# First two heads of a fused attention and MLP kernel: the ranking of head 1 before score 0, one inverse for three tiles, v of head 0 later

## What is computed

```python
q_assign = np.argmax(np.einsum('bhsd,hcd->bhsc', q_n, c_n), axis=-1)
k_assign = np.argmax(np.einsum('bhsd,hcd->bhsc', k_n, c_n), axis=-1)
mask = q_assign[:, :, :, None] == k_assign[:, :, None, :]
scores = np.where(mask, scale * np.matmul(q, k.transpose(0, 1, 3, 2)), -1000000000.0)
attn = np.exp(scores - np.max(scores, axis=-1, keepdims=True))
attn = attn / (np.sum(attn, axis=-1, keepdims=True) + 1e-09)
x = np.matmul(attn, v)
...
g = P / (Q + 1e-06)
x2 = g @ w_out
...
out = silu(x2 @ w_gate) * (x2 @ w_val) @ w_out
```

## Time and profile before

| what | value |
|---|---|
| median of 3 runs | 784.21 us (783.18 to 785.2) |
| the profiled execution's own time | 783.12 us |
| its span in the profile | 781.4 us, so 1.72 us lie around it |
| PE busy | 775.7 us (99%) |
| DVE, ACT, POOL busy | 569.3, 514.9, 524.8 us |
| DMA queue of SP and ACT (q1) | 27.0% of 16 engines |

### The profile page before, as it was taken

The page is one execution under the profiler, slowest core; times in us unless marked ns, Lnnn a source line. Parts: engine busy times, 40 slices in busy tenths (PEclk is TensorE's granted clock), DMA queues, the critical chain, the costliest instruction groups (busy, mean ns, idle before and its releaser), DMA issues.

```text
span 781.4 us, 12694 instructions
## 1 busy us (share of the span) xinstructions
PE 775.7 (99%) x4239; PEld 702.2 (90%) x4239; DVE 569.3 (73%) x1046; ACT 514.9 (66%) x958; POOL 524.8 (67%) x459
## 2 busy tenths in 40 slices
PE   9999999999999999999999999999999999999998
PEld 9999999999998888888888888899999999999997
DVE  6999999999996888777776877654544555554454
ACT  5888888888886787777768789554544444333322
POOL 6778999998585898212222488879888975665620
PEclk9999999999999999999999999999999999999999
DMA  8775674644302600000000011342111204211002
GB/s 196 172 189 147 173 175 120 162 120 117 85 29 82 189 0 1 1 0 1 1 0 1 28 30 53 87 131 54 48 34 55 55 27 136 55 37 46 27 1 81
DMA packets 57521, 57.53 MB, mean 74 GB/s; under 512 B 6576, under 2 KB 44272, under 8 KB 57456
## 3 DMA queue, kind: packets, MB, share of 16 engines
q1 hardware_dynamic: 57216, 56.13, 27.0%
q10 hardware_dynamic: 240, 0.59, 0.3%
HBM read 33.59 MB, written 3.15 MB: 47 GB/s over the span
## 4 chain that ended last, share of the span: by engine, by line
PE 98%; DVE 1%; ACT 0%; issue 0%; POOL 0%; ACTq 0%; POOLq 0%
PE ps L1247 19%; PE ps L1249 19%; PE ps L1248 19%; PE ps L1399 8%; PE ps L1416 4%; PE ps L1343 4%; PE ps L1344 4%; PE ps L1342 4%; PE ps L1418 4%; PE ps L1380 4%; PE ps L1385 4%; PE ps L1450 3%; PE ps L1243 1%; DVE probT_lo L1169 0%; PE ps L1354 0%; DVE neg_max L1143 0%
## 5 line engine op out<-in xcount | busy, mean ns | idle before, releaser
L570 POOL TENSOR_TENSOR den<-den,mag 128x512 f32<-128x512 f32 x48 | 62.3, 1298 | 122.0 <-ACT den L759 121.8
L629 POOL TENSOR_TENSOR w_lo<-w_raw,w_hi 128x768 fp32r<-128x768 f32 (+1 forms) x48 | 101.7, 2127 | 56.4 <-ACT w_hi L812 56.4
L1249 PE MATMUL ps<-x_hi,w_lo 128*128 128x512 f32 (+1 forms) x384 | 139.4, 363 | 0.0
L1247 PE MATMUL ps<-x_hi,w_hi 128*128 128x512 f32 (+1 forms) x384 | 139.1, 362 | 0.0
L1248 PE MATMUL ps<-x_lo,w_hi 128*128 128x512 f32 (+1 forms) x384 | 139.1, 362 | 0.0
L656 POOL TENSOR_SCALAR prob<-prob,row_inv 128x768 f32<-128x768 f32 x96 | 85.6, 907 | 29.3 <-DVE row_inv L1159 28.2
L1169 DVE TENSOR_TENSOR probT_lo<-ps,probT_hi 128x384 fp32r<-128x384 f32 x192 | 97.5, 549 | 6.5 <-ACT probT_hi L900 5.5
L900 ACT ACTIVATE probT_hi<-ps 128x384 fp32r<-128x384 f32 x192 | 83.7, 488 | 26.1 <-PE ps L1399 24.9
L1143 DVE TENSOR_REDUCE neg_max<-ps 128x1 f32<-128x768 f32 x96 | 90.9, 948 | 1.0 <-PE ps L1385 0.8
L880 ACT ACTIVATE prob<-ps,neg_max 128x768 f32<-128x768 f32 x96 | 86.7, 903 | 1.5 <-DVE neg_max L1143 1.2
L1399 PE MATMUL ps<-ident,prob 128*128 128x128 f32 x576 | 80.1, 275 | 1.3 <-DVE probT_lo L1169 1.1
(11 more groups left out here) (150 smaller groups left out, 1994.3 us busy)
## 6 DMA issues: line engine op xcount, KB each, us to landing
w_raw<-in_moe_w_gate SPq DMA_DIRECT2D x48, 128.0 KB, 2.3
w_raw<-in_moe_w_val SPq DMA_DIRECT2D x48, 128.0 KB, 2.6
k_hihi<-qk_hi SPq DMA_DIRECT2D x31, 192.0 KB, 4.0
w_raw<-in_moe_w_in SPq DMA_DIRECT2D x16, 256.0 KB, 3.6
w_raw<-in_moe_w_out SPq DMA_DIRECT2D x16, 256.0 KB, 4.9
qk_raw<-in_q SPq DMA_DIRECT2D x16, 192.0 KB, 3.3
qk_low<-qk_hi SPq DMA_DIRECT2D x16, 192.0 KB, 4.4
v_raw<-in_v SPq DMA_DIRECT2D x16, 192.0 KB, 2.6
```

The source lines that it names most:

```text
L629: did(g.tensor_tensor(lo[:, wave, :], raw[:, wave, :], hi[:, wave, :].bitcast(F32), ALU.subtract), s_w2lo)
L1247: mm(dst, hi, m_hi, start=start, stop=False)
L1249: return mm(dst, lo, m_hi, start=False, stop=stop)
```

## The change

Head 1's table now has both groups of logits at steps -10 and -9, the sum, the largest and the marks at -8 and -7, the transposed marks at -6, and rank and cluster rows at -5, all ahead of score 0 at step 0. `marks_at` needs no exception for head 1 any more, and ACT's cluster rows of head 0 (L956) go behind the copy of head 1's marks (they now stand at the step of head 1's cluster rows, -5). SP's order of DMAs is the same but for v of head 0, which is loaded behind the six small DMAs of head 1's cluster rows. POOL splits it at step 5 in place of -4; the low part of head 3 moves from step 5 to 4. `den_at` has no single tiles any more: the three tiles of the first half get one sum and one reciprocal, at step 3, behind the marks of head 2 (`last`). The zeros behind head 0's marks go from 5 to 4; the 4 and 7 beside head 1's logits go, and 3 come behind head 1's transposed marks; ahead of score 4 there are 2, not 3; ahead of turn 1 there are 2, not 4.

```diff
--- before.py
+++ after.py
@@ -266,12 +266,12 @@
     STAGES = (0, 2, 8, 8, 8, 8, 10, 10, 11, 11)
     FIRST = {S_LOGIT_0: -12, S_LOGIT_1: -11, S_SUM: -10, S_TOP: -10, S_MARKS: -9, S_TOPT: -8, S_RANK: -7, S_CLUSTER: -6}
     FOURTH = {S_LOGIT_0: 6, S_LOGIT_1: 7}
-    SECOND = {S_LOGIT_0: -10, S_LOGIT_1: -7, S_SUM: -6, S_TOP: -6, S_MARKS: -5, S_TOPT: 1, S_RANK: 2, S_CLUSTER: 2}
+    SECOND = {S_LOGIT_0: -10, S_LOGIT_1: -9, S_SUM: -8, S_TOP: -8, S_MARKS: -7, S_TOPT: -6, S_RANK: -5, S_CLUSTER: -5}
     THIRD = {S_SPLIT: -5, S_LOGIT_0: 2, S_LOGIT_1: 3, S_SUM: 3, S_TOP: 3, S_MARKS: 3, S_TOPT: 4, S_RANK: 5, S_CLUSTER: 6}
-    FIRST_V, FIRST_W1, LOW_AT = -4, 5, {3: 5, 4: 9}
-    FIRST_DEN, FIRST_T, FIRST_PV = 2, 4, 8
-    WARM_CEN, WARM_CENT, WARM_LOGIT, WARM_MARKS, WARM_TOP, WARM_ROWS, WARM_TILE = 19, 6, 4, 4, 5, 7, 3
-    WARM_TURN, WARM_RANK = 4, 2
+    FIRST_V, FIRST_W1, LOW_AT = 5, 5, {3: 4, 4: 9}
+    FIRST_T, FIRST_PV = 4, 8
+    WARM_CEN, WARM_CENT, WARM_LOGIT, WARM_TOP, WARM_NEXT, WARM_TILE = 19, 6, 4, 4, 3, 2
+    WARM_TURN, WARM_RANK = 2, 2
     STEPS = range(FIRST_STEP, NT + PV_LAG + HALF + 1)
 
     def head_at(step, stage):
@@ -303,7 +303,7 @@
 
     def marks_at(step):
 
-        return 1 if step == 0 else head_at(step, S_RANK) if head_at(step, S_RANK) != 1 else None
+        return head_at(step, S_RANK)
 
     def turn_at(step):
 
@@ -313,10 +313,8 @@
 
     def den_at(step):
 
-        if FIRST_DEN <= step < FIRST_DEN + HALF:
-            return 0, slice(step - FIRST_DEN, step - FIRST_DEN + 1)
         half = (step - HALF) // HALF
-        if (step - HALF) % HALF == 0 and 1 <= half < NG:
+        if (step - HALF) % HALF == 0 and 0 <= half < NG:
             return half, slice(half % 2 * HALF, half % 2 * HALF + HALF)
         return None, None
 
@@ -457,11 +455,11 @@
             load_qk(1)
             load_qk(2)
             copy_hi(0, hi_copies(0))
-            load_v(0)
             load_qk(3)
             copy_hi(1, hi_copies(1))
             copy_lo(1)
             send_cluster(1)
+            load_v(0)
             load_qk(4)
             copy_hi(2, hi_copies(2))
             copy_lo(2)
@@ -651,7 +649,7 @@
             for step in STEPS:
                 half, cols = den_at(step)
                 if half is not None:
-                    pool.wait_ge(s_inv, HALF + half if half else cols.stop)
+                    pool.wait_ge(s_inv, half + 1)
                     for i in range(cols.start, cols.stop):
                         did(g.tensor_scalar(prob[i][:, :], prob[i][:, :], row_inv[:, i:i + 1], 1.0,
                                         ALU.mult, ALU.mult), s_norm)
@@ -676,7 +674,7 @@
                     if step == when:
                         split_low(h)
 
-                h = (step - V_STEP) // T if step > 0 else 0
+                h = (step - V_STEP) // T if step >= T else 0
                 if step == (T * h + V_STEP if h else FIRST_V) and h < NH:
                     pool.wait_ge(s_v_in[h % 2], 16 * (h // 2 + 1))
                     if h >= 2:
@@ -950,7 +948,7 @@
                 h = early_at(step, S_SUM)
                 if h is not None:
                     copy_low(h)
-                if early_at(step, S_CLUSTER) == 0:
+                if early_at(step, S_CLUSTER) == 1:
 
                     sc.wait_ge(s_row0, 2)
                     s.activation(qk_low[0][0:C, 0, :].rearrange("c (t n) -> c t n", t=T)[:, 1:T, :],
@@ -1147,15 +1145,14 @@
                 half, cols = den_at(step)
                 if half is not None:
 
-                    n = HALF + half if half else cols.stop
                     if half >= 2:
                         ve.wait_ge(s_norm, HALF * (half - 1))
                     else:
                         ve.wait_ge(s_eps, 1)
-                    ve.wait_ge(s_exp, HALF * (half + 1) if half else cols.stop)
+                    ve.wait_ge(s_exp, HALF * (half + 1))
                     v_.tensor_reduce(row_den[:, cols], row_sum[:, cols, :], AX.X, ALU.add
                                      ).then_inc(s_den, 1)
-                    ve.wait_ge(s_den, n)
+                    ve.wait_ge(s_den, half + 1)
                     v_.reciprocal(row_inv[:, cols], row_den[:, cols]).then_inc(s_inv, 1)
 
             def low_parts(step):
@@ -1193,7 +1190,8 @@
                     marks(h)
                 maximum(step)
                 late = step >= 2 * T and step % T == HALF
-                if not late:
+                last = step == HALF
+                if not late and not last:
                     inverses(step)
                 if products_first(step):
                     x_sum(step)
@@ -1218,6 +1216,8 @@
                 h = early_at(step, S_MARKS)
                 if h is not None:
                     marks(h)
+                if last:
+                    inverses(step)
                 if step == 4 * T:
                     ve.wait_ge(s_par_in, 32)
                     v_.tensor_scalar(a_neg, a_raw, -1.0, None, ALU.mult)
@@ -1354,8 +1354,8 @@
                     last = transpose(ps[0:T * C, PREP, n * P:(n + 1) * P],
                                      is_top[:, n, :, :].rearrange("p t c -> p (t c)"), ident[:, :])
                 last.then_inc(s_topT, 1)
-                if h == 0:
-                    warm(WARM_TOP)
+                if h < 2:
+                    warm((WARM_TOP, WARM_NEXT)[h])
 
             def scores(step):
                 i = tile_at(step)
@@ -1454,10 +1454,6 @@
                     last.then_inc(s_logit, 1)
                     if h == 0:
                         warm(WARM_LOGIT)
-                    elif h == 1:
-                        warm(WARM_ROWS)
-                elif h == 1:
-                    warm(WARM_MARKS)
 
             pe.wait_ge(s_zeros, 1)
             warm(WARM_CEN)
```

## The result

| | before | after |
|---|---|---|
| median | 783.99 us (783.18 to 785.75, 17 runs) | 785.49 us (784.41 to 787.46, 17 runs) |
| profiled execution, its span | 783.12, 781.4 us | 785.49, 783.7 us |
| start of turn 0, start of turn 2 on PE | 19.44, 23.52 us | 22.23, 26.04 us |

The account below looks back on a forecast made before the run. PE's own work and idle moments were taken as the bound. Turn 0's 1.42 us delay, partly regained by turn 1, left turn 2 and the end +1.2 late; added to the median 784.21, this gave 785.4 us, range 783.5 to 787.0.

Parts of the forecast that it names:

- the range: Span given for the changed kernel's measured time: 783.5 to 787.0 us.
- the step that carried it: One sum behind head 2's marks makes turn 0 wait for POOL's norm: 20.86 in place of 19.44, 1.42 us late.
- the 784.21 of three runs: Median of before's runs shown to the forecaster, 1.1 us above the profiled execution; the forecast time starts from it.
- Three inverses in one: At turn 0 on PE: start at 20.86 in place of 19.44, 1.42 us late, with PE idle for 2.0 us.
- Turns 1 and 2: On PE: turn 1 at 22.68, 0.97 us late; turn 2 at 24.75, 1.2 us late.
- Nothing comes back: From turn 2 on, ACT, DVE and POOL are all late by the same; nothing shrinks, so the end moves one for one.
- Head 0's rank and score 0 at 13.25: Early on PE: head 0's rank at 11.38 instead of 11.28, score 0 starting near 13.25.
- v at no cost: Head 0's v loaded and split later costs nothing: split done by 26.3, first product with v at 29.0.
- Head 1's move hidden: Head 1's rank ahead of score 0 hides in score 1's wait for ACT's rows; score 3 is 0.23 us early.
- The wait for ACT's rows at score 1: Score 1 must wait for ACT's cluster rows at 14.17 and starts at 14.25, where it was 14.20.
- The bounds 0 to +0.4, 1.2 to 1.6 and 0 to 0.5 back: Limits for the early part, turn 0's added wait, and what turns 1 and 2 return; summed as +0.7 to +1.8.
- The clock: Slower rival: PE's clock falls in the idle gap before turn 0, +2.2 on top of 1.2, 787.6 us; chance 0.12.

Follow-up runs that it names:

- a_oldv: The changed kernel with v of head 0 loaded and split early again: 784.42 us, before beside it 783.45.
- a_fill: The changed kernel with fourteen products of zeros ahead of turn 0, where PE otherwise stands idle: 784.52 us, before beside it 783.45.
- a_zeros: The changed kernel with four zeros put back between head 1's two groups of logits: 785.95 us, before beside it 783.76.
- b_inv3: The kernel before with only the one sum and reciprocal for three tiles, behind head 2's marks: 785.76 us, before beside it 783.76.
- a_inv1: The changed kernel with one sum and reciprocal per tile again, at steps 2, 3 and 4: 784.13 us, before beside it 783.76.
- a_invfront: The changed kernel with the one sum and reciprocal of three tiles ahead of head 2's marks on DVE: 783.53 us, before beside it 783.45.
- b_head: The kernel before with only head 1's ranking ahead of score 0 and twelve fewer zeros: 782.93 us, before beside it 783.45.
- b_v: The kernel before with only head 0's v loaded late and split at step 5, head 3's low part at step 4: 785.06 us, before beside it 783.76.
- b_v_2: The same kernel as b_v run once more, on another chip than the other experiments: 784.28 us, before beside it 783.58.
- b_head_2: The same kernel as b_head run once more: 783.06 us, before beside it 783.65.
- a_q3late: The kernel a_inv1 with head 3's q and k loads issued behind head 1's high copies: 783.13 us, before beside it 783.65.
- a_front_oldv: The changed kernel with the one inverse ahead of head 2's marks and v of head 0 early: 783.22 us, before beside it 783.65.

## Why the forecast was right, and where not

Its size and its sign were right: +1.2 forecast, +1.5 in the medians, and the time inside the range. So was the step that carried it. That the number came so near is in part luck: v's cost and head 1's gain, both taken as nothing, are of like size and opposite sign, and the forecast was added to the 784.21 of three runs, which is 1.1 above before's profiled execution, while after's profiled execution is its median. From profile to profile the time rose by 785.49 - 783.12 = 2.37 us, twice the forecast.

- *Three inverses in one: right.* From head 2's second logits to turn 0 the forecast had 20.86 - 17.25 = 3.61 us; the profile after has 22.23 - 18.51 = 3.72. The idle stretch was 1.71, forecast 2.0. With the full clock up to there turn 0 stands at 21.04 in a_oldv and at 21.33 to 21.42 in a_fill, a_zeros and b_inv3. b_inv3 makes this wait alone, a_inv1 takes it away and a_invfront leaves 0.57 of it.
- *Turns 1 and 2: right.* From turn 0 to 1 the forecast had 1.82, measured 1.87; from 1 to 2 2.07, measured 1.94.
- *Nothing comes back: right.* In all fourteen profiles the span is turn 2's start, plus the idle time by issue, plus 757.2 to 757.9 us. The page's 98% on PE had said so.
- *Head 0's rank and score 0 at 13.25: wrong by 0.4 to 0.6.* At the full clock score 0 stood at 13.83 in a_fill and 13.69 in a_inv1, and score 3 at 16.88 and 16.74 in place of 16.44. This is most of the 0.5 us by which turn 0 missed 20.86. Where head 1's logits could begin early (b_head, last section) score 0 stood at 12.95.
- *v at no cost: wrong.* This is the step that failed. The forecast followed v itself, whose lateness did cost nothing (POOL's split stood at 25.71, forecast 24.5, and no turn waited for it), and called the gain on the queue one without a taker. It did not ask what moves up in v's place. Head 3's loads did, and the last copy ahead of score 0 landed 0.5 to 0.6 later in b_v and b_v_2 than in before. Price: a wait of 0.2 to 0.3 at score 0, +0.4 to +0.5 at turn 2, +0.7 and +1.3 in the two medians, both clear of 1. A part of this lies ahead of the wait, and in b_v 1.2 us of the profile are the idle moment at 51 us; what of it is v's isn't shown.
- *Head 1's move hidden: mis-sized.* It was taken as +0.10 and then -0.23 at score 3, with no effect. It is worth about -0.5 by itself, for single inverses leave turn 0 free to follow score 4: 18.56 and 19.12 for 19.44. No interval shows this by itself. The wait for ACT's rows at score 1 that the forecast hid the move in "was there before as well" by its words, but in before PE goes from score 0 to score 1 in 14.20 - 13.49 = 0.71 us and the view of waits has no wait for `qk_low`; in b_head there is none either.
- *Two slips.* The bounds 0 to +0.4, 1.2 to 1.6 and 0 to 0.5 back add up to +0.7 to +2.0, not +1.8, and the zeros that went are twelve, not seven. Neither changes the forecast; a_zeros, with four of them back, has turn 2 at 25.23, a_fill without them at 25.15.
- *The clock: too small a chance, and a size that held.* It had 0.12 and +2.2 us. The kernels with an unfilled stretch of 1.7 us (after, a_zeros, a_oldv, b_inv3) had a low clock in 22 of 45 executions, all others but before in 15 of 99, before in none of 104. In after such executions are 786.27 on average and the others 785.05. So it adds about 0.6 to after's mean. That the share falls from 9 of 17 to 2 of 11 when the stretch is filled speaks for the stretch, but the counts are small, and they don't tell a fall in the stretch from one ahead of 12 us. The stretch doesn't decide alone: after, a_zeros and b_inv3 have the same 1.7 us and the same transposes behind it as a_oldv, and their profiles keep the full clock there. A fall in the stretch costs 2.5, one ahead of 12 us some 0.85, as after's turn 2 of 26.04 against 25.15 and 25.23 says. That second place was not in the forecast at all.

By turn 2 at the full clock the parts are: one inverse behind the marks +1.6 to +1.8, v late +0.4 to +0.5, head 1 ahead -0.2 to -0.7. Together, at 25.15 to 25.23, they are +1.6 to +1.7, and the clock comes on top. All of this is measured from before's one profile, and b_head's two profiles lie 0.5 apart, so the two smaller parts are no larger than that scatter. Undisturbed executions of after are 1.1 above before's median, not 1.6; where before's other executions lose what its profiled one doesn't isn't shown.

What stays open: why the clock falls ahead of 12 us in some executions. It is not the four zeros between head 1's logits; whether the others that went matter (seven behind head 1's logits are gone, and there are fewer behind head 0's marks and ahead of score 4) wasn't tried by itself. b_head, which lacks them all, had 1 and 2 of 11.

## What to carry to other kernels

Where a result is pooled over several tiles, what counts is where the pooled instruction stands in its engine's order: behind a chain that comes from another engine it takes over that chain's lateness, and one place earlier it cost nothing that the medians here show. When a DMA leaves an early place in a queue, look at what moves up into it before calling the move free. When differences are under 1 us, look at a late milestone and the tail behind it apart, and at more than one profile of the same kernel.

## What the runs showed of the hardware

*Idle moments by issue.* In six of the fourteen profiles PE has idle time at single scores that is put down to no other engine, 0.5 to 1.5 us in all. In the waits of PE's weight loads, a_inv1 has 1.5 us in three pieces:

```profile
PEld ps L1380 <- issue: 1.5, 3, 0.7
```

They stand at 78.69, 107.35 and 121.93 us in a_inv1, at 91.97 in b_head, 94.11 in a_zeros, 94.30 and 122.86 in b_inv3, near 51 in both profiles of b_v. The same kernel run again, b_head_2, has none, nor have before and after. a_inv1's profiled execution, 784.60, is 0.5 above its own median, so its other executions seem to have less of it. What these moments are no run here shows.

*DVE and POOL side by side.* DVE's low part of head 1 (two inputs of 128x768) ran 1.62 us in a_inv1 beside a copy of POOL that took 0.83. In b_head the same two, begun 0.1 to 0.2 us earlier, took 1.02 and 1.65. The rows of DVE and POOL, of b_head and then of a_inv1:

```profile
7.55 1.02 DVE L1010 SCALAR_TENSOR_TENSOR qk_lo<-qk_raw,q_scale,qk_hi 128x768 fp32r<-128x768 f32 x1 [0.70 <-ACT qk_hi L943]
7.61 1.65 POOL L648 TENSOR_SCALAR k_hihi<-qk_hi 64x768 fp32r<-64x768 f32 x1
```

```profile
7.72 1.62 DVE L1010 SCALAR_TENSOR_TENSOR qk_lo<-qk_raw,q_scale,qk_hi 128x768 fp32r<-128x768 f32 x1 [0.79 <-ACT qk_hi L943]
7.71 0.83 POOL L648 TENSOR_SCALAR k_hihi<-qk_hi 64x768 fp32r<-64x768 f32 x1
```

DVE began at 7.55 in b_head, ahead of POOL's 7.61, and at 7.72 in a_inv1, behind POOL's 7.71. So it is in the other profiles: where DVE is 0.06 to 0.10 ahead (b_head, a_q3late, a_front_oldv) POOL's copy takes 1.61 to 1.65, and where POOL is ahead it takes 0.83 and DVE 1.19 to 1.62, the less the later DVE begins. Only b_v_2 has DVE 0.02 ahead (7.60 to 7.62) and DVE at 1.66. The Trainium skill, "GPSIMD Engine Reference", section "Specifications", says that the two share their interface to SBUF when a DVE instruction has two inputs there, and these rows agree. It decides when head 1's logits begin: with head 1 ahead and no zeros between its logits, head 0's transposes stand at 9.91 to 9.98 in the three profiles with DVE first, and at 10.64 to 10.85 in the six with POOL first. b_head and b_head_2, one kernel, lie on either side (9.98 and 10.64), so it differs from one execution to the next.
